# GpSimd's share of the weight preparation, reordered in a fused FFT and two-layer-pair kernel

## The reference

```python
X = fft(fft(x, axis=1), axis=2).real          # x: (2, 3008, 256), float32
x = X.reshape(6016, 256)
h = x @ w_in1;  r = max(h, 0);  g = r * r     # w_in1: (256, 2048)
z = g @ w_out1                                # w_out1: (2048, 256)
h = z @ w_in2
P = a0 + a1*h + a2*h^2 + a3*h^3
Q = 1 + |b0|*|h| + |b1|*h^2
out = (P / (Q + 1e-6)) @ w_out2               # float32 throughout
```

## Time and profile before

| | us |
|---|---|
| median of three runs | 1026.41 |
| lowest, highest | 1025.45, 1027.29 |
| the profiled execution, its time | 1025.84 |
| its span | 1024.0 |
| TensorE busy in the span | 997.3 (97%) |
| VectorE busy | 945.6 (92%) |
| ScalarE busy | 905.5 (88%) |
| GpSimd busy | 582.4 (57%) |

### The profile page before, as it was taken

The page is one execution under the profiler, slowest core; times in us unless marked ns, Lnnn a source line. Parts: engine busy times, 40 slices in busy tenths (PEclk is TensorE's granted clock), DMA queues, the critical chain, the costliest instruction groups (busy, mean ns, idle before and its releaser), DMA issues.

```text
span 1024.0 us, 13742 instructions
## 1 busy us (share of the span) xinstructions
PE 997.3 (97%) x5096; PEld 844.7 (82%) x5096; DVE 945.6 (92%) x1035; ACT 905.5 (88%) x935; POOL 582.4 (57%) x310
## 2 busy tenths in 40 slices
PE   9989989999999999999999999999999999999887
PEld 8788878888888888888888888888888888888776
DVE  2358899999999999999999999999999999999898
ACT  2348889999999999999999999999999999899796
POOL 0054955556566565565665655656656556556375
PEclk9999999999999999999999999999999999999999
DMA  8875000001001001001001001001001000000000
GB/s 236 309 238 182 25 1 27 1 1 47 1 1 47 1 1 47 1 1 47 1 1 47 1 1 47 1 1 46 1 1 37 5 1 22 1 21 1 0 21 16
DMA packets 25918, 38.02 MB, mean 37 GB/s; under 512 B 1806, under 2 KB 19098, under 8 KB 25722
## 3 DMA queue, kind: packets, MB, share of 16 engines
q1 hardware_dynamic: 25804, 37.14, 11.5%
q10 hardware_dynamic: 48, 0.02, 0.0%
HBM read 25.31 MB, written 11.84 MB: 36 GB/s over the span
## 4 chain that ended last, share of the span: by engine, by line
DVE 45%; PE 43%; issue 10%; ACT 1%; POOL 1%; DVEq 0%; ACTq 0%; POOLq 0%
PE ps L926 20%; PE ps L917 10%; DVE den_s L766 7%; DVE den_s L777 7%; DVE den_s L779 7%; DVE g_value L767 6%; DVE g_value L787 6%; DVE g_value L759 3%; PE ps L942 3%; PE ps L954 3%; DVE g_value L760 3%; PE ps L860 3%; DVE ps L731 3%; PE ps L884 2%; PE ps L871 1%
## 5 line engine op out<-in xcount | busy, mean ns | idle before, releaser
L926 PE MATMUL ps<-g_hi,w_out_lo 128*128 128x512 f32 (+1 forms) x764 | 298.3, 390 | 5.5 <-POOL w_in_lo L528 3.1
L926 PE MATMUL ps<-g_hi,w_out_hi 128*128 128x512 f32 (+1 forms) x764 | 298.5, 391 | 0.0
L926 PE MATMUL ps<-g_lo,w_out_hi 128*128 128x512 f32 (+1 forms) x728 | 283.2, 389 | 0.0
L526 POOL CAST g_hi<-g_value 128x1024 fp32r<-128x1024 f32 x86 | 89.4, 1040 | 334.9 <-DVE g_value L787 334.9
L528 POOL TENSOR_TENSOR g_lo<-g_value,g_hi 128x1024 fp32r<-128x1024 f32 x86 | 208.0, 2418 | 6.9
L519 POOL TENSOR_TENSOR g_lo<-g_value,g_hi 128x1024 fp32r<-128x1024 f32 (+1 forms) x86 | 203.6, 2367 | 0.0
L926 PEld LDWEIGHTS ps<-g_hi,w_out_lo 128*128 128x128 f32 x764 | 144.5, 189 | 33.6 <-POOL w_in_lo L528 4.0
L926 PEld LDWEIGHTS ps<-g_hi,w_out_hi 128*128 128x128 f32 x764 | 143.9, 188 | 29.0
L926 PEld LDWEIGHTS ps<-g_lo,w_out_hi 128*128 128x128 f32 x728 | 137.4, 189 | 25.5
L766 DVE SCALAR_TENSOR_TENSOR den_s<-den_s,b_abs,ps 128x1024 f32<-128x1024 f32 x88 | 112.4, 1277 | 6.1 <-ACT g_value L607 4.8
L917 PE MATMUL ps<-z_hi,w_in_lo 128*128 128x512 f32 x352 | 111.2, 397 | 6.4 <-DVE g_value L769 6.4
(11 more groups left out here) (121 smaller groups left out, 1901.1 us busy)
## 6 DMA issues: line engine op xcount, KB each, us to landing
x_s<-x SPq DMA_DIRECT2D x15, 384.0 KB, 5.4
out_t<-out_s SPq DMA_DIRECT2D x11, 512.0 KB, 6.1
w_out_unsplit_lo<-w_out SPq DMA_DIRECT2D x2, 2048.0 KB, 14.4
tw_s<-twiddle SPq DMA_DIRECT2D x1, 3012.0 KB, 15.8
y_hi_dram<-y_stage_hi SPq DMA_DIRECT2D x10, 256.0 KB, 5.4
y_lo_dram<-y_stage_lo SPq DMA_DIRECT2D x10, 256.0 KB, 6.0
w_in_raw<-w_in SPq DMA_DIRECT2D x4, 512.0 KB, 7.3
w_in_unsplit_lo<-w_in SPq DMA_DIRECT2D x4, 512.0 KB, 6.1
```

The costliest lines, as they stand in the source:

```text
L926: last = nc.tensor.matmul(acc[:, mb, 0:n], w[a][:, f, mb * P:(mb + 1) * P], g[c][:, i, 0:n], start=(f == 0 and j == 0), stop=(f == FB - 1 ...
```

## The change

GpSimd waits for the stored middle row and clears it first, then splits `w_out1`. The low part of each chunk of the second weights waits in addition until VectorE has made so many low parts of its own: `dve_lo1` of 4 to 7 for the four chunks of `w_in2`, of 8 to 10 for the first three of `w_out2`. The fourth chunk of `w_out2` is split behind `keep_lo1(10)`, with no such wait. `w2_ready` becomes two semaphores, and TensorE's waits name the one or the other with the same chunk. `warm_s` shrinks from four blocks of 128 columns to one, which the warm-up matmuls read four times.

```diff
+W2_AFTER = 4
-            warm_s = s1_s[:, 0, 0:4, :]
+            warm_s = s1_s[:, 0, 0:1, :]
...
-            def split(hi, lo, chunk, ready):
+            def split(hi, lo, chunk, ready, units=0):
                 written = counted(nc.gpsimd.tensor_copy(hi, chunk))
                 pool.wait_ge(w_step, written)
+                after(pool, dve_lo1, units)
                 nc.gpsimd.tensor_tensor(lo, chunk, hi.bitcast(F32), ALU.subtract).then_inc(ready, 1)
...
-            pool.wait_ge(w_out1_loaded, 16)
-            split_out(w_out1_s, w_out1_raw, w_out1_ready)
             pool.wait_ge(w_row_stored, 32)
             for w in w_in1_s:
                 pool.memset(w[0:1, 1, :].bitcast(F32), 0.0).then_inc(mid_row_zeroed, 1)
+            pool.wait_ge(w_out1_loaded, 16)
+            for c in range(FB // W_BLOCKS):
+                split_out(c, w_out1_s, w_out1_raw, w_out1_ready)
...
-                split(w_in2_s[0][:, :, cols], w_in2_s[1][:, :, cols], w_in2_raw[:, :, cols], w2_ready)
+                split(w_in2_s[0][:, :, cols], w_in2_s[1][:, :, cols], w_in2_raw[:, :, cols], w_in2_ready, W2_AFTER + c)
             pool.wait_ge(w_out2_loaded, 16)
-            split_out(w_out2_s, w_out2_raw, w2_ready)
+            for c in range(FB // W_BLOCKS - 1):
+                split_out(c, w_out2_s, w_out2_raw, w_out2_ready, W2_AFTER + DFF // W_COLS + c)
...
             for s in range(HEAD, STEPS):
                 if s > SKEW:
                     split2(s - SKEW - 1)
                 keep_lo1(s)
+                if s == HEAD:
+                    split_out(FB // W_BLOCKS - 1, w_out2_s, w_out2_raw, w_out2_ready)
...
-                nc.tensor.matmul(ps[:, 0, :], warm_s[:, 0, :], warm_s, start=True, stop=True)
+                nc.tensor.matmul(ps[:, 0, :], warm_s[:, 0, :], warm_s.to_broadcast([P, 4, P]), start=True, stop=True)
...
-                        pe.wait_ge(w2_ready, second * 2 * P // W_COLS + 1)
+                        pe.wait_ge(w_in2_ready, second * 2 * P // W_COLS + 1)
...
-                        pe.wait_ge(w2_ready, DFF // W_COLS + multiplied * 2 // W_BLOCKS + 1)
+                        pe.wait_ge(w_out2_ready, multiplied * 2 // W_BLOCKS + 1)
```

More of the change, by code:

```diff
@@ L221, in fft_moe_kernel @@
         w_in1_loaded = [sem(f"w_in1_loaded{n}") for n in range(DFF // W_COLS)]
-        w_step, w_out1_ready, w2_ready = sem("w_step"), sem("w_out1_ready"), sem("w2_ready")
+        w_step, w_out1_ready, w_in2_ready, w_out2_ready = (
+            sem(n) for n in ("w_step", "w_out1_ready", "w_in2_ready", "w_out2_ready"))
         w_row_stored, w_rows_loaded, mid_row_zeroed = sem("w_row_stored"), sem("w_rows_loaded"), sem("mid_row_zeroed")
@@ L485, in counted, with split_out @@
                 return steps[0]
-            def split(hi, lo, chunk, ready):
+            def split(hi, lo, chunk, ready, units=0):
                 written = counted(nc.gpsimd.tensor_copy(hi, chunk))
                 pool.wait_ge(w_step, written)
+                after(pool, dve_lo1, units)
                 nc.gpsimd.tensor_tensor(lo, chunk, hi.bitcast(F32), ALU.subtract).then_inc(ready, 1)
[L493 to L496, removed]
-            pool.wait_ge(w_out1_loaded, 16)
-            split_out(w_out1_s, w_out1_raw, w_out1_ready)
+            def split_out(c, dst, raw, ready, units=0):
+                rows = slice(c * W_BLOCKS, (c + 1) * W_BLOCKS)
+                split(dst[0][:, rows, :], dst[1][:, rows, :], raw[:, rows, :], ready, units)
             pool.wait_ge(w_row_stored, 32)
```

## The result

The changed kernel took 1024.76 us in the median of 16 runs (1023.77 to 1027.65), the kernel before 1026.39 in 16 runs beside it (1025.16 to 1028.11). The ratio is 0.9984, with a 95% interval of 0.9976 to 0.9991: a real gain, of 1.6 us in the medians, and less than the 0.2% named ahead. Forecast were a gain of 1.2 us and a median of 1025.2. The profiled execution took 1024.83 us, its span is 1023.0, against 1025.84 and 1024.0 before.

The account below looks back on a forecast made before the run. TensorE (97% busy) and VectorE (92%) were taken to bound the kernel. Terms -0.3 - 1.8 + 0 + 0.9 = -1.2 us took the profiled 1025.84 to 1024.6, as a median 1025.2; range 1023.2 to 1026.9.

Parts of the forecast that it names:

- Warm-up memset: At the kernel's start: memset of 128 instead of 512 columns saves 0.3 us, bounds 0 to 0.36.
- Middle row: Before the first down1: clearing the row first removes TensorE's 2.90 us wait, worth 1.8 us, bounds 1.5 to 2.9.
- Waits for VectorE's low parts: GpSimd's second-weight splits: the added waits are open when reached, cost 0; bounds 1.0 us gained or lost.
- The lockstep: Second-weight splits: CAST, subtraction and VectorE low part take turns, 4.48 us against TensorE's 4.25; forecast to stay.
- Fourth chunk: Before the fourth up2: moved w_out2 subtraction holds VectorE's first reciprocal, 0.9 us later, bounds 0 to 2.4.
- Sum: Whole kernel: -0.3 - 1.8 + 0 + 0.9 = -1.2 us, median 1025.2 us; forecast's chance 0.50.
- the seam: Where the transform phase ends and step 0 begins; clearing the middle row first was to gain 1.8 us there.
- A: Rival, whole kernel: more gained, no collision or looser lockstep, 1023.3 to 1024.3 us; chance 0.28.
- the collision: First reciprocal (L777): it meets the moved fourth chunk's subtraction on GpSimd and waits, 0.9 us later.
- clock piece: Part of A, at 145.05 us: if TensorE's clock stays up behind its wait, up to 1.8 us more gained.
- B: Rival: transfer ScalarE awaits at 65.56 stays put, memset gives nothing; -1.5 + 0.9 = -0.6, 1025.8 us; chance 0.13.
- C: Rival, following steps: GpSimd put back holds L777 longer, 4.7 us over twelve steps, net +3.5, 1029.9 us; chance 0.09.

Follow-up runs that it names:

- d1: Kernel before with one edit, the warm-up block of 128 columns read four times: 1026.25 us, ratio 0.9995.
- d2: Kernel before with one edit, the fourth chunk of w_out2 split behind keep_lo1(10): 1026.74 us, ratio 1.0002.
- c3: Changed kernel without the waits of the second weights' low parts for VectorE's count: 1024.66 us, ratio 0.9985 to the kernel before.
- d3: Changed kernel with the second weights' low parts set to zero by memset, not computed: 1022.81 us, ratio 0.9960 to the kernel before.
- c1: The changed kernel run again, nothing altered, beside the kernel before: 1024.55 us, ratio 0.9981.
- c4: Changed kernel with the fourth chunk of w_out2 split directly behind the third again: 1023.81 us, ratio 0.9978 to the kernel before.
- d4: c4 with the w_in2 loads issued behind the stores of tiles 5 to 8, not 1 to 4: 1022.85 us, ratio 0.9962 to the kernel before.

## Why the prediction was right, point by point

**Warm-up memset, -0.3.** This step failed, though its size is inside the bounds named. The memset saved its 0.3 us, but "TensorE is then busy without a gap" overlooked that the memsets of before stand behind the landing of `w_out1`, and that the warm-up matmuls scatter by 1.25 us. d1 gives 0.7 in the medians with an interval that holds zero, and nothing at the first `down1` (77.61 for 77.47). I take it for 0.

**Middle row, -1.8.** Right: what comes next was the low part of tile 7 behind a landing, and then the outer product, in that order. On the mean of seven and three profiles the first addition moved by 1.8 us (1.64 and 0.3 of the warm-up were forecast for it), the first `down1` by 2.2. TensorE kept 2.4 GHz through the two short waits (0.6 to 1.4 us) in all seven; in the three with the late memset the granted clock fell to 0.50 to 0.54 over some 2 us between 66 and 70, and the first `down1` came up to 0.6 us behind the low part that it needs (d2). With the early memset it starts as soon as that low part is done: TensorE lost its lead, as written. `w_out1`, split by 64.9 us, held nobody.

**Waits for VectorE's low parts, 0.** Right: c3. The lockstep goes on with and without them. Its price, put at four times 0.25, is 0.9 to 1.3 us by d3, and the groups that it stretches are four or five. That goes with how long after the start of VectorE's fourth low part GpSimd begins on `w_in2`: 1.73 us in the first profile of the changed kernel (five groups), 1.35 in c1 and 1.37 before (four each).

**Fourth chunk, +0.9.** Right to a tenth, in size and place: the reciprocal at 2.12 us (about 2.1 forecast), 0.90 us in the stretch from the first to the fourth `up2`, 0.7 in the medians of c1 and c4. The time of d2 doesn't show it by itself.

**Sum.** Part of the fit is luck: the 0.3 of the warm-up is not there, and the seam gave more than its 1.8. At the first `up2` the changed kernel and c1 to c4 are 2.0 us earlier than the kernel before, d1 and d2 (mean 115.31 for 117.35); less 0.9 that is 1.1. The medians say 1.6 and 1.8. The difference of some 0.6 us is within the intervals (0.9 to 2.5 us gained in the first), and what makes it up stays open. One candidate is TensorE's clock further on: over whole runs it was granted at 0.9967 in the mean in c1 and at 0.9945 in the kernel before beside it. No run tests that.

**Rivals.** A's two main pieces didn't come: the collision took place and the lockstep stayed. Its clock piece exists, but as scatter between executions of one kernel. B's landing does vary, by more than the 0.3 that B took, and to both sides. C didn't come: the second reciprocal takes 1.29 us in the chain, against 1.31 before.

## What to carry to other kernels

When a wait is taken away, look in the timeline for what the next instruction on each engine would still wait for; here the 2.9 us wait hid a landing and an outer product, and was worth about 2. Work that is moved to an idle engine is to be laid, with its start and end, beside the instructions of the engine that the traces show it holding up, here VectorE's with two inputs in SBUF: the moved chunk gave back 0.9 us, nearly half of the gain, and leaving it where it was is free. And where a landing is what comes next, the order of the transfers (d4) is worth more than another reordering of the engines.

## What the runs showed of the hardware that was not expected

- TensorE's clock behind one and the same wait of 2.41 to 2.46 us fell to 1.2 GHz in seven of thirteen profiles and stayed at 2.4 GHz in six. Where it fell, the next twelve matmuls took 4.43 to 4.58 us instead of 2.7 to 2.8.
- Where GpSimd and VectorE start within 0.03 us, the recorded starts don't tell who is held: at 115.26 and 115.29 (the changed kernel) GpSimd's CAST was the one held (2.13 us), at 116.11 and 116.14 (c3) it was VectorE (2.09), with the CAST recorded 0.03 ahead in both.
- A start 0.8 us earlier at stage 1 was down to 0.1 us at 48.8, where GpSimd waits for a load: `w_out1` landed at 48.35 in d1, 48.46 before and 48.88 in d2, with stage 1 started at 5.20, 6.00 and 6.74.
